# A gated recurrence and an expert MLP on one core: six units open at the front of TensorE's queue, and other places for the work that feeds them

## The reference

```python
sig = 1.0 / (1.0 + np.exp(-f_logit))
f = lower_bound[None, None, :] + (1.0 - lower_bound[None, None, :]) * sig
i = 1.0 - f
for t in range(S):
    h = f[:, t] * h + i[:, t] * x[:, t]
    y[:, t] = h
...
h = x @ w_in                      # x: the states y, 12160 tokens x 256; w_in 256 x 2048
relu6 = np.clip(h + 3.0, 0.0, 6.0)
g = h * relu6 / 6.0
return (g @ w_out).astype(np.float32)   # w_out 2048 x 256
```

## Time and profile before

| | |
|---|---|
| median of the runs | 1001.95 us |
| profiled execution, its own time | 1002.81 us |
| its span, first to last instruction | 1000.6 us |
| PE busy | 988.0 us, 99% |
| DVE busy | 826.9 us, 83% |
| ACT busy | 711.1 us, 71% |
| POOL busy | 202.8 us, 20% |
| mean granted TensorE clock | 0.997 |

### The profile page before, as it was taken

How to read it: one execution, slowest core, us unless ns; L and a number is a source line. 1 busy time by engine, 2 the same in 40 slices (tenths; PEclk the granted TensorE clock), 3 DMA queues, 4 the chain that set the end, 5 groups by cost and what they waited for, 6 DMA issues and landing times.

```text
span 1000.6 us, 12922 instructions
## 1 busy us (share of the span) xinstructions
PE 988.0 (99%) x4372; PEld 820.3 (82%) x4372; DVE 826.9 (83%) x1186; ACT 711.1 (71%) x1208; POOL 202.8 (20%) x142
## 2 busy tenths in 40 slices
PE   7999999999999999999999999999999999999998
PEld 6887888888888888888888888888888888888886
DVE  6999898888888888788788789788878878886765
ACT  5666777777767777777776777777777677677665
POOL 2435033104013111211300311311121040131000
PEclk8999999999999999999999999999999999999999
DMA  7203011102101010110110210011011021000001
GB/s 247 79 1 102 22 32 54 61 2 64 43 22 30 33 64 22 43 64 11 54 48 16 64 43 22 22 43 64 21 43 64 1 64 43 1 1 14 29 1 43
DMA packets 13793, 42.38 MB, mean 42 GB/s; under 512 B 1440, under 2 KB 2208, under 8 KB 13728
## 3 DMA queue, kind: packets, MB, share of 16 engines
q1 hardware_dynamic: 13728, 41.56, 12.3%
HBM read 29.10 MB, written 12.45 MB: 42 GB/s over the span
## 4 chain that ended last, share of the span: by engine, by line
PE 94%; DVE 4%; issue 1%; ACT 1%; DMA 0%; SPq 0%; DVEq 0%
PE y_ps L941 16%; PE y_ps L942 16%; PE y_ps L943 16%; PE x_ps L923 8%; PE x_ps L924 8%; PE x_ps L925 8%; PE v_ps L923 4%; PE v_ps L924 4%; PE v_ps L925 4%; PE z_ps L924 2%; PE z_ps L923 2%; PE z_ps L925 2%; PE y_ps L906 1%; PE y_ps L908 1%; PE y_ps L907 1%
## 5 line engine op out<-in xcount | busy, mean ns | idle before, releaser
L705 DVE TENSOR_TENSOR g_lo<-g,g_hi 128x512 fp32r<-128x512 f32 (+1 forms) x352 | 272.2, 773 | 45.4 <-ACT g_hi L490 44.5
L941 PE MATMUL y_ps<-g_hi,w_out_hi 128*128 128x512 f32 (+1 forms) x704 | 274.0, 389 | 0.0
L942 PE MATMUL y_ps<-g_lo,w_out_hi 128*128 128x512 f32 (+1 forms) x704 | 273.2, 388 | 0.0
L943 PE MATMUL y_ps<-g_hi,w_out_lo 128*128 128x512 f32 (+1 forms) x704 | 273.2, 388 | 0.0
L490 ACT CAST g_hi<-g 128x512 fp32r<-128x512 f32 (+1 forms) x352 | 209.0, 620 | 17.2 <-DVE g L700 16.9
L941 PEld LDWEIGHTS y_ps<-g_hi,w_out_hi 128*128 128x128 f32 x704 | 132.1, 188 | 29.0 <-ACT y_sb L500 2.3
L943 PEld LDWEIGHTS y_ps<-g_hi,w_out_lo 128*128 128x128 f32 x704 | 132.1, 188 | 26.9
L942 PEld LDWEIGHTS y_ps<-g_lo,w_out_hi 128*128 128x128 f32 x704 | 132.2, 188 | 26.4
L481 ACT ACTIVATE g<-z_ps,half 128x512 f32<-128x512 f32 (+1 forms) x88 | 60.5, 687 | 57.8 <-DVE z_ps L683 56.6
L481 ACT ACTIVATE g<-v_ps,half 128x512 f32<-128x512 f32 (+1 forms) x88 | 60.4, 686 | 55.9 <-DVE v_ps L695 55.9
L689 DVE TENSOR_TENSOR h_sb<-v_ps,h_sb 128x512 f32<-128x512 f32 (+1 forms) x88 | 60.6, 689 | 34.8 <-PE v_ps L925 33.4
(11 more groups left out here) (150 smaller groups left out, 1843.0 us busy)
## 6 DMA issues: line engine op xcount, KB each, us to landing
z_sb<-in_z SPq DMA_DIRECT2D x21, 512.0 KB, 3.5
x_sb<-in_x SPq DMA_DIRECT2D x21, 512.0 KB, 4.4
out_y<-y_sb SPq DMA_DIRECT2D x9, 1024.0 KB, 4.2
w_out_raw<-in_w_out SPq DMA_DIRECT2D x8, 256.0 KB, 7.5
w_in_raw<-in_w_in SPq DMA_DIRECT2D x6, 256.0 KB, 6.9
out_y<-y_sb SPq DMA_DIRECT2D x2, 512.0 KB, 3.0
z_sb<-in_z SPq DMA_DIRECT2D x2, 480.0 KB, 4.2
x_sb<-in_x SPq DMA_DIRECT2D x2, 480.0 KB, 4.4
```

Of the source, the lines that this page charges most:

```text
L705: nc.vector.tensor_tensor(g_lo[:, u, 0:n], g[:, u, 0:n], g_hi[:, u, 0:n].bitcast(F32), ALU.subtract).then_inc(g_lo_ready[u], 1)
L941: nc.tensor.matmul(out, w_out_hi[:, f, at], g_hi[:, u, 0:n], start=opens, stop=False)
L942: nc.tensor.matmul(out, w_out_hi[:, f, at], g_lo[:, u, 0:n], start=False, stop=False)
L943: return nc.tensor.matmul(out, w_out_lo[:, f, at], g_hi[:, u, 0:n], start=False, stop=closes)
```

## The change

On PE, six units instead of four (FRONT = 6) are opened before the first down product; units 4 and 5 use the two banks of `y_ps` that the head's second part needs only later. `head_up` becomes one pass of one unit and one k, and waits for just what that pass reads: hi·hi for the two rounded parts, hi·lo for the operand's rest, lo·hi for the weights' rest. The front's passes are ordered by that. Up to unit 15 the down product runs six units behind, at v = 16 three of them are done in a row, and from there it is four behind again.

For the first part of the head, the factor of the recurrence is made on ACT (`head_gate`, Identity with a scale for each partition and bias 1) into y_sb. A constant tile `one` is added for it. `lb` is loaded through ACT's queue; in SP's, x comes right behind z for each k, and w_in's block 2 ahead of w_out's block 0. POOL no longer makes the rests of w_in's blocks 1 and 2; DVE does.

The rest is places: rounds and rests of w4, sums at units 9, 15, 16 (before 10, 12, 14), rests of the sums later and the last of them in q = 0, `rest_of_s3(0)` behind the last operand rests of span 0, unit 31's rounding behind `copy_p1(0)`, and in q = 3 the second factor of span 1 later in the block.

```diff
+FRONT = 6
-SUMS_AT = (6, 8, 10)
-SUM_ROUNDS_AT = (8, 10, 12)
-SUM_RESTS_AT = (9, 11, 20, 21, 22, 23, 24, 25)
+CONSTANTS = 4
+BOTH_HI, X_LO, W_LO = range(3)
+SUMS_AT = (5, 11, 12)
+SUM_ROUNDS_AT = (11, 12, 13)
+SUM_RESTS_AT = (19, 21, 22, 23, 25, 26, 27)
...
-        def head_bank(s, n):
-            return (x_ps[:, 0, 0:n], x_ps[:, 1, 0:n], z_ps[:, 0:n], v_ps[:, 0:n])[s]
+        def head_bank(v, n):
+            if LEAD <= v < FRONT:
+                return y_ps[:, 1, v - LEAD, 0:n]
+            return (x_ps[:, 0, 0:n], x_ps[:, 1, 0:n], z_ps[:, 0:n], v_ps[:, 0:n])[v % LEAD]
...
-                sp.dma_start(z_sb[:, k, at], z[0, :, k, at]).then_inc(head_z_loaded[k], 16)
-                if k == 0:
-                    sp.dma_start(lb_sb[:], lb).then_inc(lb_loaded, 16)
...
+            sp.dma_start(z_sb[:, 0, at], z[0, :, 0, at]).then_inc(head_z_loaded[0], 16)
+            sp.dma_start(x_sb[:, 0, at], x[0, :, 0, at]).then_inc(head_x_loaded[0], 16)
+            load_w_in(0)
+            sp.dma_start(z_sb[:, 1, at], z[0, :, 1, at]).then_inc(head_z_loaded[1], 16)
+            sp.dma_start(x_sb[:, 1, at], x[0, :, 1, at]).then_inc(head_x_loaded[1], 16)
+            load_w_in(1)
+            load_w_in(2)
...
-            rest_of_w4(1)
-            rest_of_w4(2)
...
-                if t == 0:
-                    rest_of_s3(0)
                 rest_of_op(t, S3_T3)
                 rest_of_op(t, A22_T4)
                 if t == 0:
-                    rest_of_s3(1)
-                    rest_of_s3(2)
+                    for i in range(len(GROUPS)):
+                        rest_of_s3(i)
...
+            def head_gate(k):
+                at = head_tokens(0)
+                act.wait_ge(constants_ready, CONSTANTS)
+                nc.scalar.activation(y_sb[:, k, at], z_sb[:, k, at], ACT.Identity, bias=one[:],
+                                     scale=lb_minus_one[:, k:k + 1]).then_inc(head_gate_ready, 1)
...
+            nc.scalar.dma_start(lb_sb[:], lb).then_inc(lb_loaded, 16)
             head_sig(0)
+            act.wait_ge(head_sig_ready, 1)
+            head_gate(0)
             round_w4(0)
             head_round_op(0)
             head_sig(1)
+            act.wait_ge(head_sig_ready, K)
+            head_gate(1)
...
-                if i >= 0 and i % 2 == 0 and 4 + i // 2 < BLOCKS:
-                    round_w4(4 + i // 2)
+                if v % 2 == 0 and v > 0 and 3 + v // 2 < BLOCKS:
+                    round_w4(3 + v // 2)
...
-            head_round_g(HEAD - 1)
...
                 copy_p1(q, n)
-                if q > 0:
+                if q == 0:
+                    head_round_g(HEAD - 1)
+                else:
...
                 head_drive(0, k)
-                head_gate(0, k)
                 head_scan(0, k)
-                if k == 0:
-                    rest_of_w4(0)
+                rest_of_w4(k)
                 head_rest_of_op(k)
+            rest_of_w4(2)
...
-                if j == 3 and t + 1 < TILES:
+                if j == 3 and 0 < t < TILES - 1:
                     make_gate(t + 1, 1)
...
                 rest_of_g(q, C22, n)
+                if q == 3:
+                    make_gate(1, 1)
                 gate_h(q, C21, n)
...
+                    if q == 0:
+                        rest_of_sums(BLOCKS - 1)
...
-            def head_up(v, k):
+            def head_up(v, k, part):
...
-                if v >= LEAD:
+                if v >= FRONT and k == 0:
                     pe.wait_ge(head_g_ready, v - LEAD + 1)
...
+            for part in (BOTH_HI, X_LO, W_LO):
+                for v in range(2):
+                    head_up(v, 0, part)
+            for v in range(2, FRONT):
+                for part in (BOTH_HI, X_LO):
+                    head_up(v, 0, part)
+            for part in (BOTH_HI, X_LO):
+                for v in range(2):
+                    head_up(v, 1, part)
+            for v in range(2):
+                head_up(v, 1, W_LO).then_inc(head_up_done, 1)
+            for v in range(2, FRONT):
+                head_up(v, 0, W_LO)
+                for part in (BOTH_HI, X_LO):
+                    head_up(v, 1, part)
+                head_up(v, 1, W_LO).then_inc(head_up_done, 1)
+            for v in range(FRONT, HEAD):
+                if v < F:
+                    behind = slice(v - FRONT, v - FRONT + 1)
+                elif v == F:
+                    behind = slice(v - FRONT, v - LEAD + 1)
+                else:
+                    behind = slice(v - LEAD, v - LEAD + 1)
```

More of the change, by code:

```diff
@@ L63, in build @@
         half = sb("half", [P, 1])
+        one = sb("one", [P, 1])
         carry = sb("carry", [P, B, K])
-        sb("pad", [P, ROW - (SMALL_FROM + 5 * 32) % ROW], U8)
+        sb("pad", [P, ROW - (SMALL_FROM + 6 * 32) % ROW], U8)
         w7_hi = sb("w7_hi", [P, BLOCKS, PRODUCTS, P], F32R)
@@ L519, in head_clip @@
                     act.wait_ge(head_g_lo_ready, v - LEAD + 1)
-                nc.scalar.activation(g[:, s, 0:n], head_bank(s, n), ACT.Relu, bias=half[:],
+                nc.scalar.activation(g[:, s, 0:n], head_bank(v, n), ACT.Relu, bias=half[:],
                                      scale=1.0 / 6.0).then_inc(head_clipped_ready, 1)
@@ L583, in _ @@
                     round_op(0, A22_T4)
-                if i == 19:
+                if i == 18:
                     round_s3(0)
-                if i == 26:
+                if i == 25:
                     round_s3(1)
-            head_round_g(HEAD - 1)
             for q in range(LAST + 1):
@@ L710, in _ @@
             nc.vector.memset(half[:], 0.5).then_inc(constants_ready, 1)
+            nc.vector.memset(one[:], 1.0).then_inc(constants_ready, 1)
             dve.wait_ge(lb_loaded, 16)
@@ L756, in head_scan @@
                 if p == 0:
-                    before = carry[:, 0, k:k + 1]
+                    dve.wait_ge(head_drive_ready, k + 1)
+                    gate, before = y_sb[:, k, at], carry[:, 0, k:k + 1]
                 else:
+                    gate = z_sb[:, k, at]
                     dve.wait_ge(head_state_ready, k + 1)
                     before = x_sb[:, k, HEAD_N[0] - 1:HEAD_N[0]]
-                nc.vector.tensor_tensor_scan(x_sb[:, k, at], z_sb[:, k, at], x_sb[:, k, at], before,
+                nc.vector.tensor_tensor_scan(x_sb[:, k, at], gate, x_sb[:, k, at], before,
                                              ALU.mult, ALU.add).then_inc(head_state_ready, 1)
@@ L799, in _ @@
                 i = v - LEAD
-                if v == 1:
-                    rest_of_w4(3)
-                if i >= 0 and i % 2 == 0 and 4 + i // 2 < BLOCKS:
-                    rest_of_w4(4 + i // 2)
+                if v % 2 == 1 and 3 + v // 2 < BLOCKS:
+                    rest_of_w4(3 + v // 2)
                 if i in (1, 2):
                     head_drive(1, i - 1)
-                    head_gate(1, i - 1)
+                    head_gate(i - 1)
                 if i in (3, 4):
@@ L948, in _ @@
                                  start=True, stop=True)
-            for k in range(K):
-                for v in range(LEAD):
-                    up = head_up(v, k)
-                    if k == K - 1:
-                        up.then_inc(head_up_done, 1)
-            for v in range(LEAD, HEAD):
-                for d in range(K):
-                    head_down(v - LEAD, d)
+            for part in (BOTH_HI, X_LO, W_LO):
[21 more added lines that the diff above has]
+                    behind = slice(v - LEAD, v - LEAD + 1)
+                for u in range(behind.start, behind.stop):
+                    for d in range(K):
+                        head_down(u, d)
                 for k in range(K):
-                    up = head_up(v, k)
+                    for part in (BOTH_HI, X_LO, W_LO):
+                        up = head_up(v, k, part)
                 up.then_inc(head_up_done, 1)
```

48 lines of the change are left out of this document (21 added, 27 removed).

## The result

The changed kernel takes 994.02 us (median of 993.85, 993.92, 994.33 and 994.12) against 1002.08 us (1001.84 to 1002.9): 0.9919 of before, with a 95% interval of 0.9906 to 0.9931. The forecast was 995.3 in a range of 993.2 to 998.8. The profiled execution took 993.85 us with a span of 992.1, so 8.5 of the 8.96 us between the two profiled executions are inside the span. The medians are only 8.06 us apart.

The account below looks back on a forecast made before the run. PE, busy 988.0 of 1000.6 us, bounds the kernel; the loss lies in its front. 5.7 + 1.35 - 0.1 - 0.5 + 0.5 + 0.16 = 7.1 us off 1002.81 gives 995.7, less 0.4 is 995.3; range 993.2 to 998.8.

Parts of the forecast that it names:

- The first state: Front, k = 0: x lands at 5.1 us, drive and scan end at 7.0, PE starts at about 7.7.
- The rival that x would come no earlier: Loads at the front: x no earlier (0.5 us), w_in's block 2 0.4 later; 996.6 us, chance 0.12.
- The factor on ACT: Front: ACT makes the factor in 0.57 us, hidden for k = 0 while x lands; without that cover 0.6 us more.
- The second state: Front, k = 1: with POOL's rests on DVE, 1.8 us leave the path; unit 0 complete at 12.6, before 16.1.
- T: New start of the first down product: 15.9 us, before 19.22, with 36 up matmuls done; front gains 5.7 us.
- The clock: Front: full clock taken, longest gap 1.65 us; the rival that it drops gives 998.5 us, chance 0.18.
- The wait at unit 10: At 45.76 us: PE's 1.35 us wait for unit 10's g_lo, taken as gone.
- DVE from unit 0 to 17: Head: DVE's work falls from 42.2 to 40.0 us, gate 17 starts at 53.3; 0.5 us lost, ends 0 and 2.6.
- The joint: At q = 0: PE's 0.6 us wait for copy_p1 behind unit 31's rounding goes; 0.5 us gained.
- The level of the median: Whole run: profiled execution lies 0.86 us over the median; 0.4 us taken off, 995.7 to 995.3.
- The slower rival: Front: clock falls at 7.7 us and stays at half until 24 us; 1003.9 us, chance 0.02.
- the rival of DVE as the bound: Head, around units 17 to 20: PE waits the whole 2.6 us for DVE; 997.8 us, chance 0.13.

Follow-up runs that it names:

- Each half alone: Changed kernel with only the chain to the states and the joint kept: 996.72 us; with only PE's part and the joint kept: 1000.81 us.
- PE's part alone: Changed kernel with loads, factor, rests of w4 and tables as before; six units, passes by readiness, lead of six and joint stay: 1000.81 us, ratio 0.9988.
- lb's queue: Changed kernel with lb's load back in SP's queue between z and x of k = 0: 995.36 us, ratio 0.9934.
- the chain alone: Changed kernel with four units at the front, passes unit by unit and the tables of sums, rounds and rests as before: 996.72 us, ratio 0.9947.
- the last experiment: Changed kernel with the first sums one unit later and w_out's rests of blocks 6 and 7 moved earlier on POOL: 995.31 us, ratio 0.9933.
- the experiment: Changed kernel with unit 31's rounding ahead of copy_p1(0) on ACT again: 995.35 us, ratio 0.9931.
- passes, depth and tables: Changed kernel with one undone each: passes unit by unit 995.72 us, FRONT = 4 995.83 us, old tables of sums, rounds and rests 996.67 us.

## Why the prediction was right, and where its terms were off

The mechanism was right in the main: the loss lay ahead of the first down product, the second state's chain set it before, and six units with earlier states win it back (6.5 of 8.5 us). Each half alone brings less (5.5 and 1.4 us). Where the sum came out near, some of that is offsetting misses and, for the clock, luck. The terms, by its own steps:

- *The first state.* Predicted drive 5.1, PE's first pass 7.7; measured 4.30 and 7.16. The mis-sized step is "If landing follows the issue, it lands at 5.08": lb costs x at least 1.24 to 1.29 us, not 0.46 (the drive then waits for the sigmoid, so x was there sooner still). The rival that x would come no earlier was the wrong way round. The Trainium skill, "DMA: Bandwidth & Descriptors", section "Issuing engines are not separate DMA queues", says that starting transfers from several engines saves only the sequencer's time for the start. These runs don't agree: the 1.24 to 1.29 us saved are more than the 0.46 of the sequencer.
- *The factor on ACT* took 0.76 us, not 0.57. For k = 0 it ended at 4.88, under the drive's 4.99, so it cost nothing. For k = 1 it stands on ACT ahead of the rounding of block 1, for which PE's pass at 8.93 waits; that price wasn't measured.
- *The second state.* The scan was back at 1.15 us as forecast. But it doesn't hang on where the two rests run, as the prediction had it: with them back on POOL the scan, which starts before POOL there, still takes 1.15 us. Whether the factor's move to ACT alone would have done that in the kernel before was not run.
- *T* = 15.12, not 15.9; the front's gain 6.5, not 5.7. PE came to unit 2's passes at 8.93, not 9.5, as ACT was through with the first state 0.7 us sooner; the rest is that PE then never waited. The forecast had the second state as the last thing PE waits for; it was ready before PE came.
- *The clock* was held at 1.00, as taken, but not for the reason given. The forecast took a gap of 1.65 us, from the end of the zeros at 6.05 to 7.7, and full clock across it. There was no gap: in this execution the zeros lasted until 7.32. Where PE was empty for 1.68 and 1.83 us ahead of its first pass (PE's part alone, and lb's queue), the clock of the profiled execution did fall to 0.50 behind it; in the other profiles of these experiments, with 0 to 1.46 us, it did not fall there, nor behind a gap of 1.65 us at 41.63 in the chain alone. So the forecast's gap might have gone either way, and that the clock held was partly luck.
- *The wait at unit 10* (1.35 us) is gone. Not foreseen: unit 14's up product waits 0.54 us for unit 10's gate, as a lead of six still has four banks; and down product 12 waits 0.72 us for a rest of w_out that stands behind POOL's 2.8 us operand rest. The prediction looked for such a wait at unit 6 (0.1) and there was none.
- *DVE from unit 0 to 17*: forecast 40.0 us and a gate at 53.3; measured 12.60 to 52.27, 39.7 us. (For unit 17's clip the forecast took 7.5 us off and gave no source for that number; its own terms up to there add up to 7.0.) The wait of 0.5 us put for it did not come. It was close: where DVE reached unit 17 at 53.78, in the last experiment, PE waited 0.79 us.
- *The joint*: 0.5 forecast, 0.9 by the experiment. With q = 3 and what else lies behind the mark, 1.4 us against 0.66.
- *The level of the median*: 0.4 us taken off because the profiled execution of before lay above the others; the median after lies 0.2 us over its profiled one, so the term went the wrong way by 0.6. The level of before was in part its clock (last section), which the changed kernel doesn't share.

Sum: 7.1 forecast between profiled executions, 8.96 measured. The 1.9 us missing, by stages: the front 6.5 for 5.7 (0.8 more); from there to the 512-column mark 0.6 for 1.35 - 0.1 = 1.25, as the two new waits were not foreseen (0.65 less); behind the mark 1.4 for 0.66 - 0.5 = 0.16, as DVE's wait, which was put at unit 17, did not come and the joint gave more (1.25 more); and 0.45 outside the span. Some of this cancels.

The slower rival and the rival of DVE as the bound did not occur in the changed kernel; waits for DVE at g or g_lo are what most of the undone parts ran into.

## What to carry to other kernels

When several parts of a change share one slack, undoing each alone overstates it: passes, depth and tables cost 1.7, 1.8 and 2.6 us one by one, and 2.7 together. Before a lead is made deeper, look at the engine that feeds it: its start and its extra work between units decide how much of the lead is kept. A transfer of 1 KB in rows of a few bytes is not small for what is queued behind it. And a median can be the middle between two levels: look at the granted clock of each execution before a cause is given for it.

## What was not expected of the hardware

- The kernel before spreads over 2 us (1001.1 to 1003.1 in 15 executions of one set), the changed one over 0.5 in four. The granted clock has a part in it: of 40 executions of before in the three sets, the 29 at 0.998 have a median of 1001.65 us, the 11 at 0.994 to 0.997 one of 1002.82. But those at 0.998 alone still lie from 1001.10 to 1002.92; the rest is open.
- The row of the granted clock says 1.00 from the start, but the 28 matmuls on zeros took 4.86 us in the one profile and 6.14 in the other. In the window of 4 to 5 us before there are 10 of them, after 7:

```profile
4.00:5.00 1.00, 1.00 (x7) 1.00 (x7) 0.69 (x1) 0.85 (x2) 0.00 (x0) 1.00 0.76 193
```

In both traces the zeros first start 0.21 to 0.22 us apart, a pace like that of 1.2 GHz (256 columns are 0.213 us), and then 0.12; before this changes at 3.9 us, in the changed kernel's profile at 6.9. The column doesn't show it. In the changed kernel they lasted until PE's first pass, so PE was never empty for over 0.3 us before 36 us.
- ACT took 0.76 us for the factor, whose scale and bias both come from columns in memory, and 0.58 for the sigmoid of the same size, which reads no such column. Which of the two columns costs what wasn't run.
